# Mixing attention values with the values as weights, two heads in the two column halves of TensorE, and transposed reciprocals in place of a transposed x

## What is computed

```python
# attention: keys that count are 8 global ones and the last 96 positions
scores = scale * q @ k.T + bias            # bias: slope of the head times the distance
a = np.exp(scores - max(scores)); a = a / (sum(a) + 1e-9)
x = a @ v                                  # heads side by side: (1536, 512)
# first feed-forward
h = x @ w_in                               # (1536, 1024)
solu = h * softmax(h)
y = layernorm(solu) * g_ln @ w_out         # (1536, 512)
# second feed-forward
xn = y / rms(y) * rms_g
out = (silu(xn @ w_gate) * (xn @ w_val)) @ w_down
```

## Time and profile before

| | |
|---|---|
| median of three runs | 598.04 us (596.92 to 598.3) |
| span of the profiled execution | 596.7 us |
| time of the profiled execution beside its span | not given apart |
| TensorE matmuls | 566.4 us busy, 95% of the span |
| TensorE weight loads | 511.4 us, 86% |
| VectorE | 305.0 us, 51% |
| ScalarE | 258.1 us, 43% |
| GpSimd | 74.6 us, 13% |
| mixing (L1211) | 384 matmuls, 54.2 us busy |

### The profile page before, as it was taken

One profiled execution on the slowest core, in us unless ns is written; L12 is line 12 of the kernel. 1 busy time (PEld: TensorE's weight loads), 2 busy tenths in 40 slices (PEclk: granted clock), 3 DMA queues, 4 the chain that ended last, 5 costly groups with the idle time before them and its releaser, 6 DMA issues.

```text
span 596.7 us, 10660 instructions
## 1 busy us (share of the span) xinstructions
PE 566.4 (95%) x3696; PEld 511.4 (86%) x3696; DVE 305.0 (51%) x786; ACT 258.1 (43%) x597; POOL 74.6 (13%) x215
## 2 busy tenths in 40 slices
PE   2488999999999999999999999999999999999997
PEld 1477888888888888878899999999999999999996
DVE  5478788777877898868455223222222222231211
ACT  2566756655665677646454212221222222222112
POOL 1240220222112205213010010001001000100000
PEclk9998799999999999999999999999999999999999
DMA  7676464433443343232532100010020000000000
GB/s 171 185 192 163 132 182 125 121 101 101 124 113 103 105 126 96 83 135 82 176 109 93 49 23 2 1 70 1 1 70 0 0 0 35 0 0 36 2 1 36
DMA packets 22965, 46.95 MB, mean 79 GB/s; under 512 B 4128, under 2 KB 4128, under 8 KB 22928
## 3 DMA queue, kind: packets, MB, share of 16 engines
q1 hardware_dynamic: 22928, 46.48, 26.8%
HBM read 40.18 MB, written 6.29 MB: 78 GB/s over the span
## 4 chain that ended last, share of the span: by engine, by line
PE 78%; DVE 9%; DMA 3%; issue 3%; POOL 3%; ACT 2%; SPq 1%; ACTq 0%; DVEq 0%
PE hidden L396 9%; PE hidden L397 8%; PE hidden L398 8%; PE mixed L1211 5%; PE mixed L396 3%; PE mixed L397 3%; PE scores_b L396 3%; PE scores_b L397 3%; PE scores_b L398 3%; PE mixed L398 3%; PE turned L396 3%; PE turned L397 3%; PE scores_a L397 3%; PE turned L398 3%; PE scores_a L396 3%
## 5 line engine op out<-in xcount | busy, mean ns | idle before, releaser
L708 ACT ACTIVATE act_hi<-act_sb 128x256 fp32r<-128x256 f32 x72 | 30.1, 418 | 108.7 <-DVE act_sb L1070 108.7
L1211 PEld LDWEIGHTS mixed<-v_in,probs_t 116*128 116x128 f32 x384 | 55.3, 210 | 14.5 <-ACT probs_t L659 10.8
L1211 PE MATMUL mixed<-v_in,probs_t 116*128 116x64 f32 x384 | 54.2, 289 | 9.8 <-ACT probs_t L659 9.8
L1070 DVE TENSOR_TENSOR act_sb<-mixed,silu 128x256 f32<-128x256 f32 x36 | 15.3, 425 | 93.7 <-PE mixed L398 93.1
L1070 DVE TENSOR_TENSOR act_sb<-turned,silu 128x256 f32<-128x256 f32 x36 | 15.3, 424 | 89.0 <-PE turned L398 86.5
L396 PE MATMUL hidden<-down_hi,act_hi 128*128 128x512 f32 x144 | 57.0, 396 | 0.1
L397 PE MATMUL hidden<-down_lo,act_hi 128*128 128x512 f32 x144 | 56.9, 395 | 0.0
L398 PE MATMUL hidden<-down_hi,act_lo 128*128 128x512 f32 x144 | 56.7, 394 | 0.0
L659 ACT ACTIVATE probs_t<-turned 116x512 f32<-116x512 f32 x48 | 28.7, 597 | 60.7 <-PE turned L1196 60.7
L1075 DVE TENSOR_TENSOR act_lo<-act_sb,act_hi 128x256 fp32r<-128x256 f32 x72 | 30.6, 425 | 34.9 <-ACT act_hi L708 34.9
L649 ACT ACTIVATE probs<-logits,neg_max 128x232 f32<-128x232 f32 x96 | 45.7, 482 | 5.8 <-DVE neg_max L961 5.8
(11 more groups left out here) (140 smaller groups left out, 1537.2 us busy)
## 6 DMA issues: line engine op xcount, KB each, us to landing
qk_raw<-qk_pairs SPq DMA_DIRECT2D x96, 180.0 KB, 3.5
v_in<-v_windows SPq DMA_DIRECT2D x12, 464.0 KB
staging<-w_gate SPq DMA_DIRECT2D x3, 1024.0 KB, 6.5
staging<-w_val SPq DMA_DIRECT2D x3, 1024.0 KB, 5.5
y_spill<-y_out SPq DMA_DIRECT2D x12, 256.0 KB, 8.4
staging<-w_down SPq DMA_DIRECT2D x3, 1024.0 KB, 5.5
y_in<-y_spill SPq DMA_DIRECT2D x6, 512.0 KB, 3.7
out<-o_sb SPq DMA_DIRECT2D x12, 256.0 KB, 2.1
```

Source lines behind the costliest of these rows:

```text
L708: nc.scalar.activation(act_hi[:, slot], act_sb[:, slot], ACT.Copy).then_inc(act_rounded, 1)
L1070: nc.vector.tensor_tensor(act_sb[:, slot], val_ps[slot][:, 0:WIDE], silu[:, slot], ALU.mult).then_inc(act_ready, 1)
L1211: ins = pe.matmul(mixed[:, head * d:(head + 1) * d], probs_t[:, p % 2, h, half], v_in[:, even, half, head * d:(head + 1) * d], start=(half ...
```

## The change

`mix_pair` exchanges the operands: 64 columns of `v_in` are stationary, 128 columns of `probs_t` move. The result of a head is 64 x 128 with the head's dimensions on the partitions: the even head goes to partitions 0 to 63 (the left columns of TensorE's array), the odd head to 64 to 127. The bank `mixed` so holds x transposed, without the division. The loop now goes over halves outside and heads inside.

The reciprocal belongs to a token, and the token now lies along the free dimension. `invert_sums`, in step 3 on VectorE after `take_logits`, forms denominators and reciprocals and copies each reciprocal 64 times into `recip_wide` (128 x 512). `turn_recip` transposes that in step 3 on TensorE after `turn_pair`, into `turned_x`. `copy_recip` brings it into `x` on ScalarE after `copy_turned`. `normalise_x` multiplies `mixed` with `x` into `x`. `turn_x` is gone, and `round_x` and `split_x` read `x` in SBUF. Waits of others for `turned_x` go from `xt_split` to `recip_copied`. The branch that is not taken is changed to match.

```diff
-            x = sbuf(one, "x", [P, heads, d])
+            x = sbuf(one, "x", [P, pairs, P])
+            recip_wide = sbuf(one, "recip_wide", [P, heads, d])
...
+            def copy_recip(a):
+                act.wait_ge(recip_turned, a + 1)
+                if not known(a) or a >= 1:
+                    act.wait_ge(xt_split, a)
+                nc.scalar.activation(x[:], turned_x[:].rearrange("p (c n) -> p c n", c=pairs), ACT.Copy
+                                     ).then_inc(recip_copied, 1)
+
             def round_x(t, even):
-                act.wait_ge(xt_ready, t + 1)
+                act.wait_ge(x_final, 16 * (t + 1))
...
-                nc.scalar.activation(xt_hi[:, even], turned_x[:], ACT.Copy).then_inc(xt_rounded, 1)
+                nc.scalar.activation(xt_hi[:, even], x[:], ACT.Copy).then_inc(xt_rounded, 1)
...
                     copy_turned(n, p)
+                    if p == 3 and is_tile(a):
+                        copy_recip(a)
...
-            def normalise_x(a, even):
+            def invert_sums(a, even):
                 dve.wait_ge(probs_ready, heads * (a + 1))
                 nc.vector.tensor_scalar(denom[:], exp_sum[:, even], 1e-9, None, ALU.add).then_inc(denom_steps, 1)
-                dve.wait_ge(denom_steps, 2 * a + 1)
+                dve.wait_ge(denom_steps, 3 * a + 1)
                 nc.vector.reciprocal(recip[:], denom[:]).then_inc(denom_steps, 1)
-                dve.wait_ge(denom_steps, 2 * a + 2)
+                dve.wait_ge(denom_steps, 3 * a + 2)
+                if not known(a) or a >= 1:
+                    dve.wait_ge(recip_turned, a)
+                nc.vector.tensor_copy(recip_wide[:], recip[:].unsqueeze(2).to_broadcast([P, heads, d])
+                                      ).then_inc(denom_steps, 1)
+
+            def normalise_x(a):
+                dve.wait_ge(recip_copied, a + 1)
                 dve.wait_ge(mixed_ready, pairs * (a + 1))
-                if not known(a) or a >= 1:
-                    dve.wait_ge(xt_ready, a)
-                nc.vector.tensor_tensor(x[:], mixed[:].rearrange("p (h d) -> p h d", h=heads),
-                                        recip[:].unsqueeze(2).to_broadcast([P, heads, d]),
+                nc.vector.tensor_tensor(x[:], mixed[:].rearrange("p (c n) -> p c n", c=pairs), x[:],
                                         ALU.mult).then_inc(x_ready, 1)
...
                     take_logits(n + 1, 1 - even if p < pairs - 1 else even, (p + 1) % pairs)
+                    if p == 3 and is_tile(a):
+                        invert_sums(a, 1 - even)
...
-                for h in range(2):
-                    head = 2 * p + h
-                    for half in range(2):
-                        ins = pe.matmul(mixed[:, head * d:(head + 1) * d], probs_t[:, p % 2, h, half],
-                                        v_in[:, even, half, head * d:(head + 1) * d],
+                for half in range(2):
+                    for h in range(2):
+                        head = 2 * p + h
+                        ins = pe.matmul(mixed[h * d:(h + 1) * d, p * P:(p + 1) * P],
+                                        v_in[:, even, half, head * d:(head + 1) * d], probs_t[:, p % 2, h, half],
                                         start=(half == 0), stop=(half == 1))
...
-            def turn_x(t):
-                pe.wait_ge(x_final, 16 * (t + 1))
...
-                for k in range(KM):
-                    ins = pe.transpose(turned_x[:, k * P:(k + 1) * P],
-                                       x[:].rearrange("p h d -> p (h d)")[:, k * P:(k + 1) * P], ident[:])
-                ins.then_inc(xt_ready, 1)
+            def turn_recip(a):
+
+                pe.wait_ge(denom_steps, 3 * a + 3)
...
+                for c in range(pairs):
+                    ins = pe.transpose(turned_x[:, c * P:(c + 1) * P],
+                                       recip_wide[:, 2 * c:2 * c + 2].rearrange("p h d -> p (h d)"), ident[:])
+                ins.then_inc(recip_turned, 1)
...
                     turn_pair(n, p)
-                    if p == 0:
-                        turn_x(t)
+                    if p == 3 and is_tile(a):
+                        turn_recip(a)
```

More of the change, by code:

```diff
@@ L61, in fused_kernel @@
     assert 2 * d == P and model == BANK and N1 == 2 and K1 == N1 * KJ and KM == KJ and HALF * 2 == WIN
-    x_general = nc.dram_tensor("x_general", (tiles, P, model), F32, kind="Internal").ap()
+    x_general = nc.dram_tensor("x_general", (tiles, P, pairs * P), F32, kind="Internal").ap()
     y_dram = nc.dram_tensor("y_spill", (tiles, P, model), F32, kind="Internal").ap()
@@ L144, in fused_kernel @@
                       "part": seq * P, "dist": seq * P, "logits": seq * P, "probs": seq * P,
-                      "probs_t": seq * P, "x": d, "slope": 1, "neg_max": 1, "sum": 1, "denom": 1, "recip": 1}
+                      "probs_t": seq * P, "x": P, "slope": 1, "neg_max": 1, "sum": 1, "denom": 1, "recip": 1}
             gen, at = {}, 0
@@ L227, in fused_kernel @@
         denom_steps = sem("denom_steps")
+        recip_turned = sem("recip_turned")
+        recip_copied = sem("recip_copied")
         x_ready = sem("x_ready")
@@ L238, in fused_kernel @@
         gen_probs_ready = sem("gen_probs_ready")
+        gen_scaled = sem("gen_scaled")
         gen_turned = sem("gen_turned")
@@ L923, in attend_tile @@
                     dve.wait_ge(gen_steps, at + 9)
+                    nc.vector.tensor_scalar(gen["probs"], gen["probs"], gen["recip"], None, ALU.mult
+                                            ).then_inc(gen_scaled, 1)
                     dve.wait_ge(gen_mixed, c + 1)
[L925 to L926 removed]
+                    nc.vector.tensor_copy(gen["x"][0:d], mixed[0:d, 0:P]).then_inc(gen_x_ready, 1)
                     dve.wait_ge(gen_x_ready, c + 1)
@@ L979, in split_x @@
                 dve.wait_ge(xt_rounded, t + 1)
-                nc.vector.tensor_tensor(xt_lo[:, even], turned_x[:].rearrange("p (k n) -> p k n", k=KM),
-                                        xt_hi[:, even].bitcast(F32), ALU.subtract).then_inc(xt_split, 1)
+                nc.vector.tensor_tensor(xt_lo[:, even], x[:], xt_hi[:, even].bitcast(F32), ALU.subtract
+                                        ).then_inc(xt_split, 1)
             def max_hidden(t, n):
@@ L1082, in one_tile @@
                     if p == 0 and is_tile(t):
-                        normalise_x(t, even)
+                        normalise_x(t)
                     if p == 3 and is_tile(t):
@@ L1207, in mix_pair @@
                     pe.wait_ge(x_ready, a)
[L1208 to L1212 removed]
+                for half in range(2):
[3 more added lines that the diff above has]
+                                        v_in[:, even, half, head * d:(head + 1) * d], probs_t[:, p % 2, h, half],
                                         start=(half == 0), stop=(half == 1))
                 ins.then_inc(mixed_ready, 1)
[L1216 to L1225 removed]
+            def turn_recip(a):
+                pe.wait_ge(denom_steps, 3 * a + 3)
+                if not known(a) or a >= 2:
+                    pe.wait_ge(ln_split, N1 * (a - 1))
+                elif a == 1:
+                    pe.wait_ge(recip_copied, 1)
+                for c in range(pairs):
+                    ins = pe.transpose(turned_x[:, c * P:(c + 1) * P],
+                                       recip_wide[:, 2 * c:2 * c + 2].rearrange("p h d -> p (h d)"), ident[:])
+                ins.then_inc(recip_turned, 1)
             def ffn_in(t, even, n, ks):
@@ L1273, in turn_y @@
                         pe.wait_ge(ln_split, N1 * (tiles - 1))
-                        pe.wait_ge(xt_split, tiles)
+                        pe.wait_ge(recip_copied, tiles)
                     elif known(b) and b == 1:
@@ L1322, in one_tile @@
                         mix_pair(a, 1 - even, p)
+                        if p == 3:
+                            turn_recip(a)
                         continue
@@ L1372, in attend_tile @@
                     for j in range(seq):
-                        ins = pe.matmul(mixed[:, 0:d], gen["probs_t"][:, j * P:(j + 1) * P],
-                                        gen["v"][:, j * d:(j + 1) * d], start=(j == 0), stop=(j == seq - 1))
+                        ins = pe.matmul(mixed[0:d, 0:P], gen["v"][:, j * d:(j + 1) * d],
+                                        gen["probs_t"][:, j * P:(j + 1) * P], start=(j == 0), stop=(j == seq - 1))
                     ins.then_inc(gen_mixed, 1)
```

11 lines of the change are left out of this document (5 added, 6 removed).

## The result

The changed kernel takes 605.14 us (median of four runs, 603.67 to 605.91) beside 598.17 for the kernel before (four runs): a ratio of 1.0107, 95% interval 1.0087 to 1.0127. It is slower by about 1.1%. The profiled execution has a span of 603.7 us where the one of before has 596.7.

A forecast was written before the change was run, and what follows sets the result against it. From step 3 to step 2 TensorE's chain and that of VectorE and GpSimd were taken as equally long. Nine tiles +2.5, three earlier about 0, prologue -0.5: +2.0 on the median 598.04, so 600.0 us, range 594 to 607.

The forecast's parts named there:

- rival B: Mixing: the two column halves do not overlap, so it saves nothing; 604.3 us, chance 0.2.
- Two equally long chains; one saving of four counts: Steady tile: TensorE ties with VectorE and GpSimd from step 3 to step 2; only step 2's mixing saving counts.
- the prediction's last case: If step 3's start were no longer tied to TensorE, all four mixing savings would count: -12 us.
- round_x and split_x read x from SBUF, same sizes: 0 ... POOL has none of its own changed, it only starts late: ScalarE's rounding and VectorE's split of x: reading SBUF costs 0; GpSimd's instructions are unchanged and only start late.
- The copy, 0.53 (0.46 to 0.61), paid in full: VectorE's new copy into recip_wide adds 0.53 us a tile, within a gapless stretch, whatever TensorE saves.
- s = 0.25: Saving of the new mixing for a pair: 0.25 us, from overlapping halves less a small price for the array's shape change.
- five slots: Mixing: only the second record of a head overlaps the next head's first; five slots of 0.11, 0.55 us, saving 0.34.
- My price for changing the array's shape: Emptying TensorE's array around each mixing: 0.15 us, twice a pair, 0.3.
- The sum of a tile: Steady tile: +0.53 from step 3 to step 2, -0.25 from step 2 to step 3; +0.28, nine tiles +2.5.
- `turn_recip` stops TensorE by about 0.4 a tile, off the path: Step 3: TensorE waits about 0.4 us for recip_wide; its chain still totals -0.35 against the other's +0.53.
- Prologue -0.5, first tiles 0: Four prologue mixings, two on the chain that ended last, counted half: -0.5 us; three tiles before the nine about 0 each.
- Rival C, the drain eats the overlap: Mixing: emptying the array costs more than overlap gives, losing 0.2 to 0.4 a pair; 612 to 622 us, chance 0.12.

The follow-up runs named there:

- mix_alone: Kernel before with only the mixing's operands exchanged, transposes of x kept (x in the wrong layout): 596.79 us, ratio 0.9967.
- split_from_sbuf: Kernel before, with split_x subtracting from x in SBUF instead of turned_x in PSUM (rest part wrong): 603.4 us, ratio 1.0080.
- split_from_psum: Changed kernel, with split_x subtracting from turned_x in PSUM instead of x in SBUF (rest part wrong): 600.59 us, ratio 1.0033 to the kernel before.
- no_wide_copy: Changed kernel without each tile's copy into recip_wide and the two waits ahead of it; recip_wide holds ones: 600.13 us, ratio 1.0030 to the kernel before.
- after_sums_first: Changed kernel with invert_sums issued ahead of take_logits in step 3: 597.94 us, ratio 0.9998 to the kernel before.
- before_qk_first: Kernel before with the split of q and k issued ahead of apply_norm in step 1: 596.46 us, ratio 0.9957.

## Why the prediction was right or wrong

The forecast was 600.0 us, slower by 2, with 594 to 607 as the range. The side is right and 605.14 lies in the range, but the size is off by a factor of 3.5 (7.0 us instead of 2.0), and the time fell near rival B (604.3), whose mechanism, no overlap, is not what happened.

- **Two equally long chains; one saving of four counts.** Right in what it says of the mixing: `mix_alone` leaves steps 3, 0 and 1 at 14.62 us (14.61 before) and shortens step 2 by 0.14. The reasons were not complete. The chain through GpSimd was not level with TensorE but 0.24 us longer in six of the nine tiles; I had read 0.06 from one. And beside the split of q and k, `xt_lo` held TensorE too, ahead of `ffn_in`. So the prediction's last case, in which the saving of all four mixings counts, needs more than one tie undone: with the split first, 0.22 us a tile of about 0.5 counted.
- **"round_x and split_x read x from SBUF, same sizes: 0 ... POOL has none of its own changed, it only starts late".** This is the step that failed. The duration of `split_x` is indeed the same, 0.69 us, but it now holds up GpSimd by 0.44 us in the very stretch where VectorE waits for GpSimd. `split_from_sbuf` and `split_from_psum` put it at 0.80% and 0.74%, 4.4 to 4.8 us. The hint stood in the trace of before: a Newton instruction of 0.93 us beside the same one of 0.34. The Trainium skill, page SBUF — State Buffer, section SBUF: two separate sides, says that VectorE and GpSimd share a port pair as an exclusive lock, which a VectorE instruction with two SBUF inputs takes against a GpSimd instruction that reads SBUF. The rows above agree with it (0.19 to 0.63 us). The page would have pointed at this term ahead of time; it doesn't give its size.
- **The copy, 0.53 (0.46 to 0.61), paid in full.** Paid in full is right, the size isn't: 0.34 to the next start, below my lower bound. I had it from the slope of L1028; the copy of 512 columns runs faster than that and takes 0.43 us in all. `no_wide_copy` prices it at 4.6 us, or 0.38 for each of 12 tiles. The 0.04 above 0.34 lie ahead of the copy, which waits for the reciprocal.
- **s = 0.25.** Measured 1.24 - 1.11 = 0.13 in one mixing and 0.14 in the mean of step 2. I had five slots; it is four, worth 0.45. But then 0.32 goes back: 0.08 ahead of the mixing (0.32 instead of 0.24 between starts), 0.14 behind its four slots (0.58 instead of 0.44), 0.10 at the first matmul of the scores (0.21 to the second, instead of 0.11; the 0.19 that stood there before held 0.08 of the mixing's loads). My price for changing the array's shape, 0.15 twice, was close to this; I counted only a part of it in s. The weight loads show where it goes. The loads of the mixing and the first of the scores:

```profile
199.52 0.42 PEld L1230 LDWEIGHTS mixed<-probs_t,v_in 116*64 116x64 f32 x8 [0.36 <-issue]
200.11 0.19 PEld L1202 LDWEIGHTS scores_a<-qk_hi 128*128 128x128 f32 x1 [0.17 <-issue]
```

  Before, the first load began right behind the last product's start and ran ahead of the mixing; now each change of shape has the loads stand idle first. The Trainium skill, page TensorEngine Tiling, section Key Properties, says that a change of the tiling mode drains TensorE. The trace agrees: 0.32 us for the two changes.
- **The sum of a tile.** By the measured terms steps 3, 0 and 1 grow by 0.34 + 0.44 = 0.78; the mean is 0.69. In two of the nine tiles it is 0.82 and in the others 0.63 to 0.74. A part of the rest is known: before, the multiplication waited 0.20 us for the reciprocal right ahead of it in 6 of 12 tiles, 1.2 us in all, and in the changed kernel other work lies between. Less the 0.14 of step 2, that is 0.55 a tile and 5.0 for nine, where I had 2.5.
- **`turn_recip` stops TensorE by about 0.4 a tile, off the path.** Right: 5.29 for step 3 against 4.57 - 0.12 + 0.44 = 4.89, and 4.89 is what `after_sums_first` has. Off the path it was too, with the chain as it stood.
- **Prologue -0.5, first tiles 0.** Not confirmed: +1.7 up to the step 2 at 70.60 in this pair of profiles. I counted the mixings and not the waits of the new order. TensorE in that stretch:

```profile
57.06 0.66 PE L1243 MATMUL turned_x<-ident,recip_wide 128*128 128x128 f32 x4 [1.25 <-DVE recip_wide L986]
...
61.43 0.74 PE L1230 MATMUL mixed<-probs_t,v_in 116*64 116x128 f32 x8 [1.44 <-DVE x L992]
...
63.95 0.56 PE L1202 MATMUL scores_a<-qk_hi 128*128 128x232 f32 x1 [1.78 <-DVE qk_hi L952]
```

  The delay of the scores grows from 0.7 us at 37.97 (to 38.70) to 1.3 at 48.90 and 1.7 at 68.91. How much of it the change causes stays open. `before_qk_first` has the same instructions in the same order as the kernel before up to the scores of step 1 at 62.31, and yet in its profile those start at 63.59, and the ones of 48.90 at 50.17, nearly as late as in the changed kernel (63.95 and 50.21). One pair of profiles can't settle a difference of this size in the first 70 us.
- **Rival C, the drain eats the overlap.** Its mechanism is there, 0.32 us, but 0.45 of overlap stands against it.

## What to carry to other kernels

Where two engines run side by side, an edit that moves an operand from PSUM to SBUF isn't free because its size and duration stay: look whether a VectorE instruction with two SBUF inputs now lies beside a GpSimd instruction on the chain. Where two chains are equally long, find out what a saving is worth by the chain that doesn't have it; here moving one split ahead of a wait was worth about as much as the new mixing (0.43% and 0.33%), and made the new mixing worth 0.22 us a tile instead of 0.13. Expect a next tie behind the one that you undo. Work that is new on a chain should go first into that chain's idle time: the sums, issued ahead of the logits, turned a change that cost 1.1% into one that, with the split first, gains 1.1%.

## What I had not expected of the hardware

- A GpSimd instruction on 128 x 1 numbers takes 0.63 us instead of 0.19 while VectorE runs an instruction of 0.69 us with both inputs in SBUF, and another takes 0.93 instead of 0.34 beside two such instructions of 0.63 and 0.42. With one of VectorE's two inputs in PSUM, the first of them takes 0.19.
- The matmuls of the two column halves run as two streams: eight of 128 columns take four slots of 0.11 us, and 0.45 more when both heads use one half (1.56 against 1.11). In the mixing at 199.53 two have begun by 199.60, and their order in the code doesn't matter (0.9889 against 0.9887).
- A copy whose source repeats each of 8 columns 64 times writes 512 fp32 columns in 0.43 us, where a multiplication of the same size takes 0.68.
